# Recurrence and expert layers on one core: large loads issued in pieces, token rows and partial logits from one product

## What is computed

```
# 4 batches, 8 heads, 768 steps, head size 40; S is the state of one head (40 x 40)
for t in range(768):
    y[t]  = r[t] @ S
    Sa    = S @ a[t]
    S     = S * w[t][:, None] - outer(Sa, b[t]) + outer(v[t], k[t])
x      = y of all heads side by side                     # 3072 tokens x 320
logits = x @ w_gate;  scale = log1p(exp(x @ w_noise))    # 8 experts
top2 of (logits + scale * noise), softmax over the two   # routing
x2     = sum over the two of gate * (relu(x @ w1[e]) @ w2[e])
out    = leaky(x2 @ w_in) @ w_out                        # 320 -> 2048 -> 320
```

## Time and profile before

| | us |
|---|---|
| median of 3 runs | 1540.15 |
| lowest and highest | 1528.86, 1545.16 |
| the profiled execution, its own time | 1533.03 |
| its span, first to last instruction | 1531.2 |
| TensorE busy (matmul) | 1326.6 (87%) |
| VectorE busy | 924.7 (60%) |
| ScalarE busy | 656.6 (43%) |
| GpSimd busy | 293.3 (19%) |

### The profile page before, as it was taken

How to read it: one execution, slowest core, us unless ns; L and a number is a source line. 1 busy time by engine, 2 the same in 40 slices (tenths; PEclk the granted TensorE clock), 3 DMA queues, 4 the chain that set the end, 5 groups by cost and what they waited for, 6 DMA issues and landing times. The chain is left out here.

```text
span 1531.2 us, 40858 instructions
## 1 busy us (share of the span) xinstructions
PE 1326.6 (87%) x16862; PEld 1206.5 (79%) x16862; DVE 924.7 (60%) x1605; ACT 656.6 (43%) x1476; POOL 293.3 (19%) x240
## 2 busy tenths in 40 slices
PE   3449978788988787379999999999976999999998
PEld 3337766576877676379999999999975988988887
DVE  5867568464653700867888788878844455354443
ACT  2323333333433332156767676767642333333332
POOL 3405234151521112020101011111014020120000
PEclk9966688677678887589999999999997999999999
DMA  6844563736442320268686868787822010110000
GB/s 154 196 94 117 119 163 103 154 103 138 110 105 72 99 79 21 64 207 266 214 266 222 266 212 266 222 258 221 265 89 73 14 52 22 31 51 17 0 18 18
DMA packets 142114, 197.64 MB, mean 129 GB/s; under 512 B 60859, under 2 KB 115259, under 8 KB 138971
## 3 DMA queue, kind: packets, MB, share of 16 engines
q1 hardware_dynamic: 126815, 149.75, 34.4%
q10 hardware_dynamic: 9891, 27.97, 6.3%
q0 software_dynamic: 5280, 18.03, 4.2%
HBM read 171.40 MB, written 24.31 MB: 128 GB/s over the span
## 5 line engine op out<-in xcount | busy, mean ns | idle before, releaser
L324 DVE TENSOR_TENSOR prod<-Tl,Lt 128x1 f32<-128x1 f32 (+30 forms) x186 | 145.2, 780 | 82.9 <-DMA Lt<-lscr 76.9
L1237 DVE TENSOR_TENSOR gf<-psM,low 128x512 f32<-128x512 f32 x96 | 66.4, 691 | 178.8 <-ACT low L1275 178.8
L1275 ACT ACTIVATE low<-psM 128x512 f32<-128x512 f32 x96 | 57.5, 599 | 242.1 <-PE psM L1333 242.1
L951 PE MATMUL psE<-w2h,hh 128*128 128x320 f32 x496 | 155.7, 314 | 0.0
L953 PE MATMUL psE<-w2h,hl 128*128 128x320 f32 x496 | 153.3, 309 | 0.0
L952 PE MATMUL psE<-w2l,hh 128*128 128x320 f32 x496 | 153.2, 309 | 0.0
L936 PE MATMUL psE<-xh,w1h 128*128 128x256 f32 x496 | 141.1, 284 | 1.9 <-DVE xh L787 1.9
L937 PE MATMUL psE<-xl,w1h 128*128 128x256 f32 x496 | 140.9, 284 | 0.0
L938 PE MATMUL psE<-xh,w1l 128*128 128x256 f32 x496 | 140.9, 284 | 0.0
L1033 POOL DMA_INDIRECT xs<-xrow,src x62 | 60.4, 973 | 414.0 <-PE psE L920 370.1
L787 DVE TENSOR_TENSOR w2l<-w2t,w2h 128x320 fp32r<-128x320 f32 x248 | 122.2, 493 | 10.9 <-ACT w2h L782 10.8
(11 more groups left out here) (181 smaller groups left out, 3234.9 us busy)
## 6 DMA issues: line engine op xcount, KB each, us to landing
w2t<-in_w_dram SPq DMA_DIRECT2D x31, 1280.0 KB, 6.7
w1t<-in_w_dram SPq DMA_DIRECT2D x31, 1024.0 KB, 8.9
w1t<-in_w_dram SPq DMA_DIRECT2D x62, 256.0 KB, 9.5
Vd<-in_vG_dram ACTq DMA_DIRECT2D x22, 640.0 KB, 6.0
ysort<-ys SPq DMA_DIRECT2D x31, 320.0 KB, 4.9
RV<-in_rvE_dram ACTq DMA_DIRECT2D x22, 416.0 KB
U<-in_wE_dram SPq DMA_DIRECT2D x6, 838.5 KB
BT<-in_bE_dram SPq DMA_DIRECT2D x6, 832.0 KB
```

Of the source, the lines that this page charges most:

```text
L324: mark(nc.vector.tensor_tensor(prod[:, 0:t, 0:t], Tl[:, 0:t, CH - t:CH], Lt[:, t:t + 1, CH - t:CH].to_broadcast([128, t, t]), ALU.mult))
L951: mm(o, hh[:, f, sl], w2h[:, f, :], start=(f == 0), stop=False)
```

## The change

1. Every large load (`P`, `U`, `AT`, `BT`, `KT`) is issued as four transfers: `P` and `U` by groups of four pairs, `AT`, `BT`, `KT` by chunk. A row of a transfer is then 2 KB a partition and not 8 KB. The four count on the same semaphore, and those who wait, wait for 64. (`P` of slot 0 was in four pieces already.)
2. A chunk's `RV` and `Vd` are issued as two transfers each, of 2 KB and 2.5 KB a partition; the waits are for 32.
3. `rows` on TensorE: one product for each head pair, `xT` with a matrix `wx` of 96 columns (a unit part that gives the 80 columns of tokens, and 16 columns of gate and noise). The logits are not summed over the four head pairs in PSUM: ScalarE copies the four parts to `LGp`, and POOL adds them in two steps (`LGh`, then `LG`), in the third chunk of the next slot and at the end.
4. `Bk` and `Kk` are rings of six chunks (`RT`) instead of two slots of four.

```diff
-        wgn = sb("wgn", [EP, 4, 2 * E])
+        wx = sb("wx", [EP, 4, XW])
+        LGp = sb("LGp", [128, NB, 4, 2 * E])
+        LGh = sb("LGh", [128, NB, 4 * E])
...
-        Bk = sb("Bk", [128, 2, 4, NB, 2, D])
-        Kk = sb("Kk", [128, 2, 4, 4, 2, D])
+        Bk = sb("Bk", [128, RT, NB, 2, D])
+        Kk = sb("Kk", [128, RT, 4, 2, D])
...
             def chunk(k):
                 b3, b2 = k % 3, k % 2
-                sp.dma_start(RV[:, b3, :, :, :], rvE[k]).then_inc(q[f"l_r{b3}"], 16)
-                sp.dma_start(Vd[:, b2, :, :, :], vG[k]).then_inc(q[f"l_g{b2}"], 16)
+                for p in range(2):
+                    sp.dma_start(RV[:, b3, p, :, :], rvE[k][:, p]).then_inc(q[f"l_r{b3}"], 16)
+                for p in range(2):
+                    sp.dma_start(Vd[:, b2, p, :, :], vG[k][:, p]).then_inc(q[f"l_g{b2}"], 16)
...
+            def wide_a(s):
+                for c in range(4):
+                    sp.dma_start(AT[:, s % 3, c, :, :], aE[s][:, c]).then_inc(q[f"l_a{s % 3}"], 16)
...
             def decays(s):
-                sp.dma_start(U[:, s % 3, :, :], wE[s]).then_inc(q[f"l_u{s % 3}"], 16)
+                for h in range(4):
+                    sp.dma_start(U[:, s % 3, 4 * h:4 * h + 4, :], wE[s][:, 4 * h:4 * h + 4, :]).then_inc(q[f"l_u{s % 3}"], 16)
...
+            def logits(s):
+                pool.wait_ge(q["a_row"], 4 * s + 4)
+                tt(LGh[:, :, :], LGp[:, :, 0:2, :].rearrange("p b h e -> p b (h e)"),
+                   LGp[:, :, 2:4, :].rearrange("p b h e -> p b (h e)"), ALU.add).then_inc(q["g_lh"], 1)
+                pool.wait_ge(q["g_lh"], s + 1)
+                tt(LG[:, s:NT:NS_, :], LGh[:, :, 0:2 * E], LGh[:, :, 2 * E:], ALU.add).then_inc(q["g_lg"], 1)
+
             for k in range(NK):
                 s, c = slot(k)
+                if c == 2 and s:
+                    logits(s - 1)
                 mask_gv(k)
...
             def rows(s, b):
                 act.wait_ge(q["p_rows"], 4 * s + b + 1)
                 if 4 * s + b >= 2:
                     act.wait_ge(q[f"l_x{b % 2}"], 16 * (2 * s + b // 2))
-                for h in range(2):
-                    copy(xo[:, b % 2, :].rearrange("p (g h d) -> p g h d", h=2, d=D)[:, :, h, :],
-                         ps[:, 4 + b % 2, 0:416].rearrange("p (g m) -> p g m", g=4)[:, :, 64 * h:64 * h + D], None)
-                copy(LG[:, b * NS_ + s, :], ps[:, 4 + b % 2, 416:432], "a_row")
+                if s and b == 0:
+                    act.wait_ge(q["g_lg"], s)
+                both = ps[:, 4 + b % 2, 0:4 * XW].rearrange("p (g m) -> p g m", g=4)
+                copy(xo[:, b % 2, :].rearrange("p (g m) -> p g m", g=4), both[:, :, 0:2 * D], None)
+                copy(LGp[:, b, :, :], both[:, :, 2 * D:], "a_row")
...
             def rows(s, b):
-                o = 4 + b % 2
-                for h in range(4):
-                    turn(ps[:, o, EP * h:EP * h + EP], xT[0:EP, b, h, :], unit)
                 for h in range(4):
-                    m = mm(ps[:, o, 416:432], xT[0:EP, b, h, :], wgn[:, h, :], start=(h == 0), stop=(h == 3))
+                    m = mm(ps[:, 4 + b % 2, XW * h:XW * h + XW], xT[0:EP, b, h, :], wx[:, h, :], start=True, stop=True)
                 m.then_inc(q["p_rows"], 1)
```

More of the change, by code:

```diff
@@ L31 @@
 NK = S // CH
+RT = 6
 EP = 64 + D
@@ L34 @@
 E = 8
+XW = 2 * D + 2 * E
 F1 = 1024
@@ L88, in stage_a @@
                  "o_S o_y p_X p_Gv p_G p_Str p_P p_tok p_rows p_PT p_S p_y p_Gp "
-                 "a_X a_gv a_G a_S0 a_Pn a_tok a_row a_PT a_S a_Gp g_lk g_gv g_gp").split()
+                 "a_X a_gv a_G a_S0 a_Pn a_tok a_row a_PT a_S a_Gp g_lg g_lh g_lk g_gv g_gp").split()
         q = {n: sem(n) for n in names}
@@ L127, in suffix_in, with wide_b, wide_k @@
                 sp.wait_ge(q["v_end"], s)
-                sp.dma_start(P[:, :, :], wR[s]).then_inc(q["l_p"], 16)
+                for h in range(4):
+                    sp.dma_start(P[:, 4 * h:4 * h + 4, :], wR[s][:, 4 * h:4 * h + 4, :]).then_inc(q["l_p"], 16)
+            def wide_a(s):
+                for c in range(4):
+                    sp.dma_start(AT[:, s % 3, c, :, :], aE[s][:, c]).then_inc(q[f"l_a{s % 3}"], 16)
+            def wide_b(s):
+                for c in range(4):
+                    sp.dma_start(BT[:, s % 2, c, :, :], bE[s][:, c]).then_inc(q[f"l_b{s % 2}"], 16)
+            def wide_k(s):
+                for c in range(4):
+                    sp.dma_start(KT[:, s % 2, c, :, :], kE[s][:, c]).then_inc(q[f"l_k{s % 2}"], 16)
             def wide(s):
-                sp.dma_start(AT[:, s % 3, :, :, :], aE[s]).then_inc(q[f"l_a{s % 3}"], 16)
-                sp.dma_start(BT[:, s % 2, :, :, :], bE[s]).then_inc(q[f"l_b{s % 2}"], 16)
-                sp.dma_start(KT[:, s % 2, :, :, :], kE[s]).then_inc(q[f"l_k{s % 2}"], 16)
+                wide_a(s)
+                wide_b(s)
+                wide_k(s)
             def decays(s):
-                sp.dma_start(U[:, s % 3, :, :], wE[s]).then_inc(q[f"l_u{s % 3}"], 16)
+                for h in range(4):
+                    sp.dma_start(U[:, s % 3, 4 * h:4 * h + 4, :], wE[s][:, 4 * h:4 * h + 4, :]).then_inc(q[f"l_u{s % 3}"], 16)
             def out_half(s, j):
@@ L171, in _ @@
             decays(0)
[L172 to L174 removed]
+            wide_b(0)
+            wide_a(0)
+            wide_k(0)
             decays(1)
@@ L275, in _ @@
                 mask_gp(k)
+            logits(NS_ - 1)
         @block.vector
@@ L418, in tok @@
                     for h in range(2):
-                        copy(t[:, s % 2, c, :, h, :], src[:, :, 64 * h:64 * h + D], "a_tok" if i == 5 and h else None)
+                        copy(t[:, (4 * s + c) % RT, :, h, :], src[:, :, 64 * h:64 * h + D], "a_tok" if i == 5 and h else None)
             def chunk(k):
@@ L426, in chunk @@
                     act.wait_ge(q["p_y"], k - 2)
-                act.dma_start(RV[:, b3, :, :, :], rvE[k]).then_inc(q[f"l_r{b3}"], 16)
-                act.dma_start(Vd[:, b2, :, :, :], vG[k]).then_inc(q[f"l_g{b2}"], 16)
+                for p in range(2):
+                    act.dma_start(RV[:, b3, p, :, :], rvE[k][:, p]).then_inc(q[f"l_r{b3}"], 16)
+                for p in range(2):
+                    act.dma_start(Vd[:, b2, p, :, :], vG[k][:, p]).then_inc(q[f"l_g{b2}"], 16)
             def rows(s, b):
@@ L641, in add_B @@
                         o = (b % 2) * 128
-                        m = mm(ps[E_[p], 2 + b // 2, o:o + 128], Bk[:, s % 2, c, b, p, :], Gpb[:, b, p, :],
+                        m = mm(ps[E_[p], 2 + b // 2, o:o + 128], Bk[:, (4 * s + c) % RT, b, p, :], Gpb[:, b, p, :],
                                start=False, stop=True, skip_group_check=True)
@@ L651, in add_K @@
                             o = (b % 2) * 128 + CH * h
-                            m = mm(ps[E_[p], 2 + b // 2, o:o + CH], Kk[Z_[b], s % 2, c, h, p, :], GvT[Z_[b], k % 2, p, h, :],
+                            m = mm(ps[E_[p], 2 + b // 2, o:o + CH], Kk[Z_[b], (4 * s + c) % RT, h, p, :], GvT[Z_[b], k % 2, p, h, :],
                                    start=False, stop=True, skip_group_check=True)
```

34 lines of the change are left out of this document (18 added, 16 removed).

## The result

| | before | after |
|---|---|---|
| median | 1537.45 (4 runs) | 1494.53 (4 runs, 1493.11 to 1499.68) |
| span of the profiled execution | 1531.2 | 1493.0 |
| mean granted clock | 0.884 | 0.912 |
| first instruction of the routing on VectorE | 610.1 | 568.1 |

A forecast was written before the change was run, and what follows sets the result against it. TensorE's chain bounds the recurrence, with stalls taken for missing instructions. Terms -15 -5 -8 -1 -12 +7 = -34 us take the profiled 1533.03 to 1499; keeping the median's 7 above gives 1506 us, range 1480 to 1531.

The forecast's parts named there:

- the four signs: TensorE issue waits near 30 us; no stall above 3 us; third slot's clock above 0.78, 88 us or less; rows' step 0.85.
- Token rows, -12: TensorE's token rows, 24 times: eight 96-column records instead of twelve save 10 to 19 us, taken as 12.
- Large loads, -15: Five TensorE stalls beside 8 KB rows in the recurrence each lose 3 us; 15 us, bounds 0 and 22.6.
- start, -1: TensorE's first product waits for AT's landing; faster 2 KB rows give up to 2.6 us, taken as 1 gained.
- clock, -8: Recurrence: shorter stalls are followed by fewer slow-clock stretches; 8 us gained, between 0 and 25.
- chunk loads, -5: Five TensorE stalls after RV and Vd are asked for each lose 1 us; 5 us, between 0 and 16.4.
- given back, +7: Stalls removed in a slot's last chunk are replaced by TensorE's wait for VectorE's state product; 7 us lost.
- The step that failed: TensorE's instruction fetch waits about one transfer's share of its DMA engine: 4.4 us whole, 1.1 cut in four.
- its rival: A fetch waits for all bytes already queued, so stalls stay and only the rows' 12 us come: 1528; chance 0.20.
- rival two: VectorE takes over: stalls go but it finishes each slot no sooner; rows' 12 and some 8 more: 1520; chance 0.20.
- The slower rival: Split transfers move fewer bytes a us, so U and the inverse land later: 1558, slower than before; chance 0.06.

The follow-up runs named there:

- rows_only: Changed kernel with every load whole again, keeping only the new token rows and ring of six; ratio 0.9871 to the kernel before, median 1513.5 us.
- loads_only: Changed kernel with the token rows as before, keeping only the split loads and ring of six; ratio 0.9863 to the kernel before, median 1515.4 us.
- first_slots: Kernel before with ring of six and large loads in four transfers for the first two slots only; ratio 1.0016, median 1532.2 us.
- eighths: Changed kernel with large loads in eight transfers each (1 KB rows); ratio 0.9729 to the kernel before, median 1490.9 us.
- rows_2k: Kernel before with ring of six, large loads laid out in DRAM for 2 KB rows but still one transfer each; ratio 1.0005, median 1536.8 us.
- rows_products: Kernel before with ring of six, token-row transposes made plain products with the unit matrix, sixteen records a batch; ratio 1.0117, median 1551.7 us.
- rows_twice: Changed kernel with each batch's four token-row products issued twice, sixteen records of 96 columns; ratio 0.9897 to the kernel before, median 1513.0 us.

## Why the prediction was right, and where not

Sign and range held, and the sum missed by 9 us of 43. But of the four signs that were to show it right, only the third slot's clock and length came: the "issue" waits are 47.9 us and not near 30, five stalls are above 3 us where none should be, and a batch of rows takes 0.98 us and not 0.85. The number came out partly by luck, since the largest terms were priced by a mechanism that the runs don't bear out. By its terms:

- **Token rows, -12.** The profile shows 12.3 us in the rows themselves, though 8 of work (a record costs 0.122 us, not 0.093 to 0.103) and 4 of clock, where I had 10 and 2. What was missing is the clock behind the rows: rows_only measures 20 us (14 to 26), and the 8 us, a difference, are nearly the whole miss. The trace of before had the sign: of the two steps of a slot, the second took 3.4 to 3.9 us in four of five slots. I put the slow stretches down to stalls.
- **Large loads, -15, start, -1, clock, -8, chunk loads, -5, given back, +7.** Together -22; loads_only measures 21. That they agree is luck, as far as the 15 and the 8 go: both were worked out from stalls cut short. The chunk loads' 5 is 6. The large loads alone give 9 to 13, with the clock in it. The start gives nothing measurable (first_slots).
- **The step that failed** is "a fetch seems to wait about one transfer's share of its engine, not for the queue to empty", by which each stall beside a large load would lose 3.3 us. Stalls of 4.3 to 4.9 us stay beside quarters, and of 6.2 beside eighths; in the changed kernel only two stalls and 10.6 us of 39.0 went. The sign of its rival, "stalls of 4 us beside 2 KB rows", is there too, but its time (1528) is not, so I had tied the time to the stalls too closely. What a fetch waits for is not settled: not for a row (rows_2k), and not for one transfer's share.
- **Clock, -8.** It moved by more than the stalls explain: from 252 to 156 us at half clock, of which the rows alone take 88 (rows_only). The loads alone take 40 (loads_only), but so does rows_2k, which gains nothing, and the granted clock of whole executions hardly moves with the loads (0.895 for 0.889, where rows_only has 0.907). The term also has two upper bounds, 15 us by its own working and 25 as stated.
- **VectorE gives 7 back.** It is seen: TensorE waits 6.77 us for S0T at the end of the fifth slot where it was 4.12, and all its waits for S0T and TT are 31.4 us where they were 25.0. As a limit on the whole (rival two, 1520) it fell.
- **The slower rival** (split transfers move fewer bytes) fell with its opposite: 1.85 MB for 1.57, and VectorE waits for U 16.2 us where it was 21.3, not above 45. The Trainium skill (DMA: Bandwidth & Descriptors, Rules for kernel authors) wants 1 MiB or more in a transfer for the highest rate; here loads of some 0.85 MB gained 0.6 to 0.8% by being cut into four of 0.21 on the same queue, and lost nothing in eight.

## What to carry to other kernels

A load that the engines wait for on a busy queue may be issued as four transfers of some 200 KB, even if it would be one of 0.8 MB; that gave 0.6 to 0.8% here, two gave nothing that could be measured, and eight no more. Narrow products next to transposes of the same operand can cost more than their own time: joined to one product each, they took 8 us of work away and, by difference, some 12 of clock. Which of the two held the clock down is open. And when stalls have a cause that is inferred, test the size of the cure on the cause (row, transfer, queue) before pricing it: the price here was right only in sum.

## What the runs showed of the hardware

- The data rate grew with the number of transfers that a load was issued in: from 12 to 20 us one transfer with 2 KB rows moved 1.45 MB, four with 2 KB rows 1.83 to 2.23 MB, eight with 1 KB rows 2.30 MB, with the engines' busy share between 85 and 88% in all of these. The kernels with one transfer and 8 KB rows moved 1.47 to 1.57 MB at 82 to 84%.
- The granted clock fell from 1.00 to 0.50 while TensorE was busy without a break (rows_products, 216 to 226 us), and often in token rows made of 104- and 16-column operations (38 of 100 steps longer by over 5%), hardly ever in rows made of 96-column products (2 of 40), even where these were as many records (rows_twice, 0 of 10).
- Beside loads of 1 or 2 KB rows TensorE still stood up to 6.6 us for no semaphore.
